# Recurrence, dense layer and routed experts in one kernel: which engine copies h, how expert pieces are buffered, and where the value products stand

## The reference, cut to what matters

```python
# recurrence, per time t
y[:, :, t] = einsum('bhd,bhde->bhe', rt, state + u * kt (outer) vt)
state = wt * state + kt (outer) vt
# dense layer, x: 3072 x 384
h = x @ w_in                      # 384 x 2048
g = h * tanh(log1p(exp(h)))
x2 = g @ w_out                    # 2048 x 384
# experts: every token goes to one of 8, the largest logits first
logits = x2 @ w_gate
out[mask_e] = maximum(x2[mask_e] @ w1[e], 0) @ w2[e]
```

## Time and profile before

| | |
|---|---|
| median of 3 runs | 844.1 us (843.27 to 844.26) |
| profiled execution | 845.52 us, its span 843.8 us |
| TensorE | 787.3 us busy, 93% of the span |
| VectorE | 649.3 us, 77% |
| ScalarE | 403.4 us, 48% |
| GpSimd | 284.9 us, 34% |
| granted TensorE clock | 0.975 of full speed on average |

### The profile page before, as it was taken

The page is one execution under the profiler, slowest core; times in us unless marked ns, Lnnn a source line. Parts: engine busy times, 40 slices in busy tenths (PEclk is TensorE's granted clock), DMA queues, the critical chain, the costliest instruction groups (busy, mean ns, idle before and its releaser), DMA issues.

```text
span 843.8 us, 16959 instructions
## 1 busy us (share of the span) xinstructions
PE 787.3 (93%) x6744; PEld 577.0 (68%) x6744; DVE 649.3 (77%) x1123; ACT 403.4 (48%) x655; POOL 284.9 (34%) x244
## 2 busy tenths in 40 slices
PE   8799999999998999999899999996799999999995
PEld 7788877777877686877677677753465665666662
DVE  8979988888979797969798897757777777766220
ACT  2457647575665757574747576920111211212221
POOL 3315362624444343344262536001212313213311
PEclk9999999999999999999999999998699999999999
DMA  9952246363554636281838262303324244235510
GB/s 311 335 197 61 73 142 246 107 212 142 179 196 139 235 98 266 76 299 58 317 101 298 86 233 91 132 20 149 138 91 179 79 156 181 98 135 206 193 41 29
DMA packets 47790, 133.48 MB, mean 158 GB/s; under 512 B 5344, under 2 KB 19808, under 8 KB 45664
## 3 DMA queue, kind: packets, MB, share of 16 engines
q1 hardware_dynamic: 38880, 93.07, 31.3%
q0 software_dynamic: 5376, 34.61, 11.1%
q10 hardware_dynamic: 3456, 4.72, 1.5%
HBM read 97.78 MB, written 34.60 MB: 157 GB/s over the span
## 4 chain that ended last, share of the span: by engine, by line
PE 35%; DVE 31%; issue 13%; ACT 12%; DMA 6%; POOL 1%; SPq 1%; DVEq 0%; ACTq 0%; POOLq 0%
PE bank L414 34%; DVE inv L925 7%; ACT t_sb L733 6%; DMA stage<-in_moe_w 5%; DVE cum L916 4%; DVE h_sb L995 3%; DVE t_sb L1002 3%; DVE stage L1023 2%; DVE kdiv L933 2%; DVE att L948 2%; ACT g_hi L733 2%; ACT L814 1%; PE bank L664 1%; DVE rdec L940 1%; ACT L822 1%
## 5 line engine op out<-in xcount | busy, mean ns | idle before, releaser
L414 PE MATMUL bank<-x_hi,win_hi 128*128 128x256 f16 x576 | 159.3, 277 | 11.6 <-DVE h_sb L995 7.6
L414 PE MATMUL bank<-x_lo,win_hi 128*128 128x256 f16 x576 | 159.0, 276 | 0.0
L414 PE MATMUL bank<-x_hi,win_lo 128*128 128x256 f16 x576 | 158.9, 276 | 0.0
L1446 POOL TENSOR_TENSOR g_lo<-t_sb,g_hi 128x512 f16<-128x512 f32 x88 | 119.8, 1384 | 87.8 <-ACT g_hi L733 87.8
L414 PE MATMUL bank<-wout_hi,g_hi 128*128 128x392 f16 (+1 forms) x416 | 129.8, 319 | 0.8 <-issue 0.8
L414 PE MATMUL bank<-wout_lo,g_hi 128*128 128x392 f16 (+1 forms) x416 | 129.6, 318 | 0.0
L414 PE MATMUL bank<-wout_hi,g_lo 128*128 128x392 f16 (+1 forms) x416 | 129.6, 319 | 0.0
L1430 POOL TENSOR_TENSOR dv<-v_tok,dot 128x384 f32<-128x384 f32 x24 | 39.6, 1649 | 203.0 <-DVE dot L955 203.0
L733 ACT ACTIVATE g_lo<-bank 128x384 f16<-128x384 f32 x64 | 31.4, 490 | 144.1 <-PE bank L414 144.1
L733 ACT ACTIVATE g_hi<-t_sb 128x512 f16<-128x512 f32 x96 | 56.0, 623 | 90.4 <-DVE t_sb L1002 86.8
L1002 DVE TENSOR_TENSOR t_sb<-t_sb,h_sb 128x512 f32<-128x512 f32 x96 | 93.4, 1001 | 6.3 <-ACT t_sb L733 4.2
(11 more groups left out here) (179 smaller groups left out, 1467.1 us busy)
## 6 DMA issues: line engine op xcount, KB each, us to landing
stage<-in_moe_w SPq DMA_DIRECT2D x32, 768.0 KB, 7.3
w_split<-stage SPq DMA_DIRECT2D x32, 768.0 KB, 5.4
wt<-in_w_turned SPq DMA_DIRECT2D x24, 258.0 KB, 6.5
kt<-in_k_turned SPq DMA_DIRECT2D x24, 256.0 KB, 6.2
rt<-in_r_turned SPq DMA_DIRECT2D x24, 256.0 KB, 6.4
r_tok<-in_r SPq DMA_DIRECT2D x24, 192.0 KB, 7.5
k_tok<-in_k SPq DMA_DIRECT2D x24, 192.0 KB, 8.5
v_tok<-in_v SPq DMA_DIRECT2D x24, 192.0 KB, 5.1
```

Of the source, the lines that this page charges most:

```text
L414: return nc.tensor.matmul(*a, **k)
L1446: G.tensor_tensor(g_lo[:, j * GW:(j + 1) * GW], t_sb[:, j * GW:(j + 1) * GW], g_hi[:, j * GW:(j + 1) * GW], ALU.subtract).then_inc(s["glo" ...
```

## The change

1. **Copies.** Odd tiles of h are copied into `h_sb` by ACT (semaphore `hca`), even ones by DVE as before. `copy_of` waits for the right one. ACT's order in a slot becomes copy, arctan of the tile before, tanh; `turn_x(n0)` (`x_hi`) goes from slot 8 to slot 7, ahead of the last arctan.
2. **Pieces.** Three input and three output buffers (`fold_w` is taken as the third). Piece n + 3 is loaded when piece n is through DVE. DVE's parts stand in slots 5, 6, 8 (and 14). Iterations 2 to 9 do three pieces each, 10 and 11 four. On SP's queue the loads for the recurrence and the pieces are interleaved in another order.
3. **Gate products.** `gated` for tiles 4 to 7 moves from slots 12 to 15 to slots 11 and 12, so that the eight stand ahead of the scan, the reciprocals, `kdiv` and `rdec` of the next chunk. `dots(n0)`, `sum_x(n0)` and `new_state(n0)` change places too.
4. **Value products.** The 12 products of `values(n)` stand singly, one behind each of the first 12 matmuls of tile 6 (chunk n0) or of sum 2 (n1), the 4 of `ktok` behind the first four of tile 7 or of sum 3. In iteration 0 and ahead of it `values` stays as it was.

```diff
+
+        def copy_of(eng, i, j):
+
+            eng.wait_ge(s["hca" if j % 2 else "hcp"], NJ // 2 * i + j // 2 + 1)
...
-            begin = [3 * (k - 2) + max(0, k - 8) for k in (i, i + 1)]
-            return range(begin[0], min(begin[1], PIECES))
-
-        SPLIT_SLOTS = (1, 3, 5, 12)
-
-        def split_now(i, slot):
-            k = SPLIT_SLOTS.index(slot)
+            begin = [3 * (k - 2) + max(0, k - 10) for k in (i, i + 1)]
+            return range(begin[0], begin[1])
+
+        def split_slots(i):
+
+            return ((1, 3, 5, 7), (2, 4, 6, 8)) if i == NI - 1 else ((1, 3, 5, 12), (5, 6, 8, 14))
+
+        def split_now(i, slot, which):
+            slots = split_slots(i)[which]
+            k = slots.index(slot) if slot in slots else PIECES
             return list(split_turns(i))[k:k + 1]
...
         def split_raw(n):
-            return stage[n % 2][:, :]
+            return (stage[0], stage[1], fold_w[0])[n % RING][:, :]
 
         def split_out(n):
-            return stage[2 + n % 2][:, :].bitcast(FP16).rearrange("p (s c) -> p s c", s=2)
+            return (stage[2], stage[3], fold_w[1])[n % RING][:, :].bitcast(FP16).rearrange("p (s c) -> p s c", s=2)
...
             def piece_in(n):
-                if n >= 2:
-                    sp.wait_ge(s["plo"], n - 1)
+                if n >= RING:
+                    sp.wait_ge(s["plo"], n - RING + 1)
+                elif n == 2:
+                    sp.wait_ge(s["fold"], 4)
                 else:
                     sp.wait_ge(s["whi"], 5 + n)
                     sp.wait_ge(s["woutlo"], 1 + n)
-                sp.dma_start(split_raw(n), piece_parts(n)[0]).then_inc(praw[n % 2], 16)
...
             def pieces_of(i, which):
                 for n in list(split_turns(i))[which]:
                     piece_out(n)
-                    if n + 2 < PIECES:
-                        piece_in(n + 2)
+                    if n + RING < PIECES:
+                        piece_in(n + RING)
...
+                if i == 1:
+                    for n in range(RING):
+                        piece_in(n)
...
+            def value_product(n, k):
+
+
+                c, q, part = n % CH, k // 3, k % 3
+                if k == 0:
+                    pe.wait_ge(s["att"], 2 * n + 2)
+                    if not first_of(n):
+                        pe.wait_ge(s["state"], with_keys(n))
+                    pe.wait_ge(s["xhi"], n)
+                    pe.wait_ge(s["xlo"], n)
+                    pe.wait_ge(ld["v"][c], 16 * (n // CH + 1))
+                if k >= 12:
+                    if last_of(n):
+                        return
+                    if k == 12:
+                        pe.wait_ge(s["ktok"], with_keys(n + 1))
+                    q = k - 12
+                    new = mm(T1[:, q * 2 * D:(q + 1) * 2 * D], ktok[:, q, :],
+                             v_tok[c][:, 2 * q:2 * q + 2, :].rearrange("p a b -> p (a b)"), start=True, stop=True)
+                    if k == 15:
+                        new.then_inc(s["u_ps"], 1)
+                elif part == 0:
+                    if not first_of(n):
+                        mm(Y[:, 2 * q * D:(2 * q + 2) * D], rdec[c][:, q, :], state[:, q, :], start=True, stop=False)
+                else:
+                    h = 2 * q + part - 1
+                    y = mm(Y[:, h * D:(h + 1) * D], att[:, h, :], v_tok[c][:, h, :],
+                           start=first_of(n), stop=first_of(n) or part == 2)
+                    if k == 11:
+                        y.then_inc(s["y_ps"], 1)
+
...
                 if j >= 3:
-                    pe.wait_ge(s["hcp"], NJ * i + j - 2)
-                elif i == 0:
+                    copy_of(pe, i, j - 3)
+                elif i >= 1:
+                    copy_of(pe, i - 1, (6, 7, 5)[j])
+                else:
                     pe.wait_ge(s["att"], 4)
...
                     for t, (a, b) in enumerate(ops):
                         last = mm(hb[HB[j]][:, f * TOK:(f + 1) * TOK], a, b, start=t == 0, stop=t == len(ops) - 1)
+                        if begin + f * len(ops) + t < end_at:
+                            value_product(values_of, begin + f * len(ops) + t)
...
             def turn(i, slot):
+                n0, n1 = CH * (i + 1), CH * (i + 1) + 1
+                between = {6: (n0, 0, 12), 7: (n0, 12, 16), 10: (n1, 0, 12), 11: (n1, 12, 16)}
+                here = between.get(slot, ()) if 1 <= i < NI - 1 else ()
                 if slot < NJ:
-                    tile(i, slot)
+                    tile(i, slot, *here)
                 elif i >= 1:
-                    sums(i - 1, slot - NJ)
+                    sums(i - 1, slot - NJ, slice(0, None), *here)
...
-                elif slot == 6:
-                    values(n0)
...
             def tanh(i, j):
-                act.wait_ge(s["hcp"], NJ * i + j + 1)
+                copy_of(act, i, j)
                 if i >= 1:
                     act.wait_ge(s["glo"], NJ * (i - 1) + j + 1)
                 A(t_sb[:, j * GW:(j + 1) * GW], h_sb[:, j * GW:(j + 1) * GW], ACT.Tanh, scale=1.0 / (SX * SW_IN)
                   ).then_inc(s["th"], 1)
+
+            def copied(i, j):
+                if j % 2 == 0:
+                    return
+                act.wait_ge(s["h"], NJ * i + j + 1)
+                if i >= 1:
+                    act.wait_ge(s["g"], NJ * (i - 1) + j + 1)
+                A(h_sb[:, j * GW:(j + 1) * GW], hb[HB[j]][:, :], scale=0.5).then_inc(s["hca"], 1)
...
                 if slot < NJ:
-                    tanh(i, slot)
+                    copied(i, slot)
                     if slot >= 1:
                         arctan(i, slot - 1)
+                    tanh(i, slot)
                     if slot == 5 and with_att:
                         keys(n0)
+                    if slot == 7 and with_att:
+                        turn_x(n0)
...
             def copied(i, j):
+                if j % 2:
+                    return
                 dve.wait_ge(s["h"], NJ * i + j + 1)
                 V.tensor_scalar(h_sb[:, j * GW:(j + 1) * GW], hb[HB[j]][:, :], 0.5, None, ALU.mult
                                 ).then_inc(s["hcp"], 1)
...
-                    if slot == 7 and with_att:
-                        sum_x(n0)
-                        new_state(n0)
...
@@ -1081,14 +1132,18 @@
                             key_side(n1)
                             masks(n0)
                         elif slot == 4:
+                            dots(n0)
                             query_side(n1)
-                        elif slot == 5:
-                            dots(n0)
-                    if slot in (3, 5, 7):
-                        if i == 1:
-                            split_piece(4 + (slot - 3) // 2)
-                        expert_piece(i, slot)
+                        elif slot == 6:
+                            sum_x(n0)
+                        elif slot == 7:
+                            new_state(n0)
+                    if slot in (3, 5, 7) and i == 1:
+                        split_piece(4 + (slot - 3) // 2)
+                    expert_piece(i, slot)
                     return
+                if slot == 8:
+                    expert_piece(i, slot)
                 if 1 <= i < NI - 1:
                     if slot == 8:
...
-                elif slot == 11 and 1 <= i < NI - 1:
-                    sum_x(n1)
-                    new_state(n1)
-                elif slot >= 12:
-                    if slot == 12 and 1 <= i < NI - 1:
+                elif slot == 11:
+                    gated(i, 4)
+                    if 1 <= i < NI - 1:
+                        sum_x(n1)
+                    gated(i, 5)
+                    if 1 <= i < NI - 1:
+                        new_state(n1)
+                elif slot == 12:
+                    gated(i, 6)
+                    gated(i, 7)
+                    if 1 <= i < NI - 1:
                         low_x(n1)
-                    gated(i, slot - 8)
+                        if with_next:
+                            products(n2)
+                elif slot >= 13:
```

More of the change, by code:

```diff
@@ L55 @@
 PIECES = 4 * E
+RING = 3
 RMAX = bass.bass_isa.ReduceOp.max
@@ L203, in moe_chain @@
         wst = [sem(f"s_wst{i}") for i in range(4)]
-        praw = [sem(f"s_praw{i}") for i in range(2)]
-        pout = [sem(f"s_pout{i}") for i in range(2)]
+        praw = [sem(f"s_praw{i}") for i in range(RING)]
+        pout = [sem(f"s_pout{i}") for i in range(RING)]
         w1g = [sem(f"s_w1g{i}") for i in range(2)]
@@ L471, in turn_x, with tile @@
                 last.then_inc(s["xT"], 1)
-            def tile(i, j):
+            def tile(i, j, values_of=None, begin=0, end_at=0):
                 if j % 2 == 0 and i == 0:
@@ L516, in last_logits, with sums @@
                 last.then_inc(s["logit"], 1)
-            def sums(i, j, part=slice(0, None)):
+            def sums(i, j, part=slice(0, None), values_of=None, begin=0, end_at=0):
                 if i == 0 and j % 2 == 0:
@@ L536, in sums @@
```

(19 more changed lines are left out.)

37 lines of the change are left out of this document (16 added, 21 removed).

## The result

The changed kernel takes 802.24 us (median of 4 runs, 798.63 to 803.10), the kernel before 844.18 us (4 runs, 843.27 to 845.98): a ratio of 0.949, with a 95% interval of 0.946 to 0.953. Forecast were 804 us.

A forecast was written before the change was run, and what follows sets the result against it. TensorE was taken to bound each iteration, stopping where VectorE, nearly as full, or a long way through ScalarE is late. Savings of 14 + 24 + 1.5 + 1 = 40.5 us from the 844.1 us median gave 804 us, range 798 to 823.

The forecast's parts named there:

- The single products: TensorE's value products standing singly hide one weight load each: 0.7 us a whole chunk, taken as 14 us in all.
- a product of 48 columns costs 0.15 in place of 0.22, one of 96 columns 0.19: TensorE's cost in us of one value product standing singly, its first weight load hidden behind the fp16 matmul.
- A: Value products on TensorE alternate with tile matmuls without gain, each waiting out both loads: 818 us; chance 0.13.
- C: No weight load overlaps where fp32 and fp16 alternate on TensorE; products cost 0.44, making it slower: 882 us; chance 0.05.
- The waits: TensorE's weight-load waits in iterations 2 to 10: 27.5 less 3.5 that stay, 24 us saved, plus 1.5 of clock.
- The allowance of 3.5 us for `att`: TensorE's short waits for the masks in iterations 2 to 10 that may stay, 0.4 us in each.
- all 9.1 us go: TensorE's ktok waits vanish because the four products needing it move behind the next tile's or sum's first matmuls.
- VectorE loses four copies: VectorE has 2.7 us less work an iteration, so TensorE's waits for n0's att and copies of h go.
- The gates in one run: Gate products moved on VectorE to where GpSimd subtracts: cost nothing, 1 us an iteration if VectorE's cover is gone.
- Rival B: VectorE becomes the bound, holding TensorE 1.5 us in each of ten iterations: 819 us; chance 0.12.
- Iterations 0, 1, 11 and the second stage: One ktok wait of 1 us goes in iterations 0 and 1; iteration 11's copies just hidden; second stage unchanged.
- rival D: ScalarE's odd copies of h become TensorE's new wait, +1.2 us an iteration: 815 us; chance 0.06.

The follow-up runs named there:

- experiment 1: The changed kernel with a chunk's value products in one run again, behind the tile or the sum: 814.8 us, ratio 0.963.
- experiment 3: The changed kernel with rings of two buffers in place of three: 854.3 us, ratio 1.012 to the kernel before.
- experiment 7: The kernel before with nothing but a ring of three buffers in place of two: 832.6 us, ratio 0.987.
- experiment 4: The kernel before with nothing but the single value products: 843.6 us, ratio 0.998.
- experiment 11: The kernel before with the single value products and the ring of three buffers: 831.8 us, ratio 0.982.
- experiment 12: The kernel before with single products, ring of three, and VectorE's pieces in turns 5, 6, 8 and 14: 824.8 us, ratio 0.976.
- experiment 5: The changed kernel with all eight copies of h on VectorE again: 803.9 us, ratio 0.952.
- Experiment 9: The changed kernel with all eight copies of h on VectorE and gate products 4 to 7 spread over the last four turns: 810.8 us, ratio 0.958.
- experiment 8: The changed kernel with the 48 gate-fold products single in iterations 0 and 1, and chunk 2's products in iteration 0: 811.4 us, ratio 0.960.

## Why the prediction was right

**The single products.** The step "a product of 48 columns costs 0.15 in place of 0.22, one of 96 columns 0.19" was measured at 0.15 and 0.20. The gain forecast for a whole chunk, 0.7 us, is 0.74 in experiment 1; for the 18 chunks of iterations 2 to 10 the working gives 12 x 0.7 + 6 x 0.6 = 12.0 us, measured are 12.5. By the mean of 0.69 for each of the other two chunks the whole term is 13.9, where 14 was taken; those two were not measured apart. Tile 6 with its 12 products takes 4.01 us (3.8 to 4.1 forecast). Rivals A and C are excluded by this, C with the whole sign: the load of an fp32 product does overlap the fp16 matmul ahead of it, although both use all rows. So what the Trainium skill (TensorE: Matmul & The Clock Gate, The mechanism) lists as the only case of overlap, a differing row group, is not the only one here: single products cost 0.15 and 0.20 us. The same section of the Trainium skill also lets a load into the background weight buffer go ahead of running matmuls; that would fit, and the prediction left it out.

**The waits.** Forecast were 27.5 us less 3.5 that stay, and 1.5 of clock: 25.5. Experiment 1 measures the sum directly, since it has the old products and no wait: 404.9 - 377.1 = 27.8 us. The allowance of 3.5 us for `att` was not needed; the clock was granted in full in all of iterations 2 to 10. The waits of the weight loads and the clock, 27.5 + 1.5 = 29 us, thus were a fair measure of TensorE's loss; its idle time alone, 20.5 us, would have been too low, since 7.3 us of the 27.8 are longer busy time (384.4 against 377.1).

**How the waits went** was named too simply. That a late load holds up `att` is shown by experiments 3 and 7: with the ring alone VectorE's wait for x_hi falls from 29.2 to 12.4 us (116 to 480 us) and TensorE's for `att` from 10.2 to 4.0. But the ring alone gave 12.6 of the 27.8 us, and "all 9.1 us go" for ktok did not come from moving the four products behind the next tile: in experiments 4 and 11, which move them, that wait rose from 8.3 to 12.5 us (116 to 480 us), and in experiment 1, which leaves them unmoved, it is gone. It went with VectorE's late pieces (experiment 12, 1.5 us left), which the prediction did not price. "VectorE loses four copies", which the prediction made the main cause for `att` of n0 and the copies, is worth 1.6 us alone; with products in one run it is worth nothing. The mechanism here was partly misread: not the amount of VectorE's work decided, but what stood ahead of the copy that TensorE needed. That 24 us came close to the 27.8 measured is in part luck, since two of the three reasons given for it do not carry it.

**The gates in one run** were taken at nothing, with up to 1 us an iteration as their price; they gave 2.1 us (366.7 - 364.6), and 5.5 where the copies are VectorE's (371.7 - 366.2). Rival B fails for the change as made: VectorE is busy for 38.04 of 41.17 us in iteration 6, and for 96% in experiment 5, and TensorE hardly waits. Experiment 9 shows how near it was: there TensorE is idle for 3.5 us.

**Iterations 0, 1, 11 and the second stage.** Ahead of iteration 2 the gain is 2.8 us, where 1 was forecast for the wait and some 1.4 is the share of iteration 1's two chunks. This term is the least certain: the mean granted clock there is 0.96 in the profile before and 0.94 in that after, over 87.0 and 84.3 us, so by an estimate from these figures 1.6 us more were lost to it after (5.1 against 3.5). Iteration 11 stays at 31.64 us with ScalarE at 28.26 (29.5 forecast), and from iteration 2 to its end TensorE waits for no copy of ScalarE, so rival D has no row. The second stage differs by 0.8 us. By its terms the span measures 12.5 + 27.8 + 2.8 + 0.8 = 43.9 us; the median fell by 41.9, forecast were 40.5.

## What to carry to other kernels

Parts of such a change don't add up: single products gave 1.3 us of iterations 2 to 10 on the kernel before and 12.5 in the changed one, since work saved on the bounding engine turns into waits while the others are just in time. So test a shortening of the bound with the waits already gone, and test a cure for waits by what stands in the queue ahead of the late instruction, not by how full its engine is. A third buffer lets the step that frees it move to a later turn; the later turns without it cost 49 us here.

## What was not expected of the hardware

In experiment 8, while fp32 products of 8 columns and fp16 tile matmuls alternated without any idle time, the granted clock stayed for 17.06 us at 0.50, the lower of the two levels (1.2 GHz) [70.75 to 87.81, above]. At full clock tile matmul and product together took 0.25 us, at the lower level 0.45:

```profile
41.80 0.27 PE L425 MATMUL bank<-x_lo,win_hi 128*128 128x256 f16 x1
41.91 0.28 PE L425 MATMUL bank<-w_gate,g_hi 128*128 128x8 f32 x2
42.05 0.27 PE L425 MATMUL bank<-x_hi,win_lo 128*128 128x256 f16 x1
```

```profile
71.66 0.37 PE L425 MATMUL bank<-x_hi,win_hi 128*128 128x256 f16 x1
71.83 0.43 PE L425 MATMUL bank<-w_gate,g_lo 128*128 128x8 f32 x2
72.11 0.37 PE L425 MATMUL bank<-x_lo,win_hi 128*128 128x256 f16 x1
```

Ahead of the falls of that kernel TensorE had stood: 1.11 and 1.10 us, for `kdiv` and `win_lo`, between 38 and 41.5 us, 2.19 us up to 55.30 and 1.88 us up to 69.51. But a pause is not needed. In the changed kernel the 48 products of 8 columns stand in four runs of 12, and the granted clock falls with the end of two of them and 1 us behind a third, at 78.8 us. At the second, two windows show TensorE busy without a pause on both sides of the fall, and the timeline the run ahead of it:

```profile
58.00:65.10 7.10, 7.10 (x66) 7.01 (x65) 4.44 (x9) 4.74 (x8) 1.69 (x1) 1.00 0.53 172
65.10:68.50 3.40, 3.40 (x18) 2.38 (x17) 2.79 (x5) 3.40 (x6) 0.00 (x0) 0.50 0.01 5
```

```profile
62.34 2.74 PE L425 MATMUL bank<-w_gate,g_lo 128*128 128x8 f32 x24
```

So a full share of busy time in the profile does not assure the full clock. Products of 48 and 96 columns that alternate with tile matmuls in iterations 2 to 10 keep a clock of 1.00. That it is the 8 columns that let it fall is likely by these rows, but no run changed the columns alone.
